# First products of two gated layers: seven products of quarter matrices instead of eight

## The chip, the cores and the metric

The kernel runs on one core of a Trainium2 chip. The time is the device time of one execution in microseconds (us), and the figure of a kernel is the median of its runs.

## What is computed

An attention over 8 batches, 8 heads, 576 positions and head size 64, whose softmaxes run over the features of q and over the positions of k, then two feed-forward layers over 4608 tokens of width 512:

```python
kv = np.einsum('bhsd,bhse->bhde', k_s, v)            # k_s: softmax over the positions
attn = np.einsum('bhsd,bhde->bhse', q_s, kv)         # q_s: softmax over the features
...
g = x @ w_gate                                       # 512 x 1536
silu = g * (1.0 / (1.0 + np.exp(-g)))
val = x @ w_val                                      # 512 x 1536
x = silu * val @ w_out                               # 1536 x 512
...
h = np.maximum(np.maximum(x @ w1, x @ w2), x @ w3)   # 512 x 768 each
out = h @ w_out                                      # 768 x 512
```

## The kernel before

Everything is float32 with a split: each operand is written as a high part in the type fp32r and the rest of it, and each product is made of three matmuls: high weights by high x, high weights by low x, low weights by high x. ScalarE makes the high part by a copy, and VectorE or GpSimd subtracts it from the original for the low part.

The 4608 tokens are nine blocks of 512. Layer 1 takes block after block, and in each the hidden width in 12 tiles of 128 (F1): a gate product into first_bank (12 matmuls of 512 columns: 4 pieces of the depth by 3), a value product into second_bank (12), and the second product of the tile before (L948 to L950, 12 matmuls), which adds up in four banks (acc_bank) over the whole block. Layer 2 has 6 tiles (F2) a block and three first products each (first_bank, second_bank, att_bank), then its second product (L965 to L967). ScalarE takes the tanh of the gate (L617) or a copy (L642), VectorE multiplies (L786, L796) or takes the maximum (L824, L830). `hidden` is then split: ScalarE writes h_hi (L556), VectorE h_lo (L693).

All weights of a layer stay in SBUF once split: 36 units of 128x512 for layer 1, read and split during the attention of batch 0 and block 0, and 24 for layer 2, during layer 1's last block. ScalarE makes the high part (L530), GpSimd the low one (L312). Apart from that GpSimd has little to do: the kv_lo split (L318) of each batch and, for batch 0, subtracting and scaling q (L325, L332).

Attention of a batch is 22 items of TensorE (ITEMS: transposed maxima KM, key-value products KV, transposed q QT, results X), each of a few matmuls into an att_bank. Batch 0 goes first; batch b + 1 is spread over block b of layer 1 by the table GAPS, one item in a gap between the 12-matmul products. VectorE does most of its elementwise work. A result goes to DRAM (x_dram) and comes back as the next blocks' x, and so do layer 1's results (x2_dram).

The order on each engine is written out by hand, and each engine takes its instructions strictly in turn; semaphores hold it where data isn't ready. Blocks in the middle run in hardware loops.

## Time and profile before

| | |
|---|---|
| median of 3 runs | 1600.42 us (1599.92 to 1603.34) |
| span of the profiled execution | 1598.4 us |
| TensorE busy | 1587.5 us, 7344 matmuls recorded |
| VectorE busy | 642.2 us |
| ScalarE busy | 399.3 us |
| GpSimd busy | 105.3 us, 115 instructions |
| DMA | 100.11 MB |

The span reaches from the first instruction to the last. A busy time is the time in which the engine had an instruction in work. A matmul's recorded duration is its latency, and the next one starts before it ends, so its cost is read from the distance of two starts. Some matmul records are missing from the trace. The layers follow each other: attention of batch 0 until about 43 us, layer 1 until about 1010 us, then layer 2.

### The profile page before, as it was taken

How to read it: one execution, taken by the hardware profiler on the slowest of the kernel's cores; microseconds unless marked ns; L12 is line 12 of the kernel's file. 1: busy time of each engine (PE TensorE's matmuls, PEld its weight loads, DVE VectorE, ACT ScalarE, POOL GpSimd, SP SyncE). 2: the span in 40 equal slices, each digit the busy share in tenths (PEclk: the TensorE clock that was granted, in tenths of full speed). 3: DMA queues.
4: the chain of work that ended last, by engine and by line, in shares of the span. 5: the costliest groups of instructions: out<-in, count | busy, mean ns of one | idle time of the engine just before them, and what ended most of it. 6: DMA issues, size and time to landing. Idle time of an engine off the chain costs nothing.

```text
span 1598.4 us, 19784 instructions
## 1 busy us (share of the span) xinstructions
PE 1587.5 (99%) x7344; PEld 1316.4 (82%) x7344; DVE 642.2 (40%) x1146; ACT 399.3 (25%) x753; POOL 105.3 (7%) x115
## 2 busy tenths in 40 slices
PE   8999999999999999999999999999999999999999
PEld 7888888888888888888888888888888888888887
DVE  6664654645645536546432322222322222222122
ACT  5543322313323223223121223211111112112111
POOL 5441000000000000000000034000000000000000
PEclk9999999999999999999999999999999999999999
DMA  8552312312223213122020032101101011010000
GB/s 232 171 149 85 100 50 82 89 61 78 62 71 90 64 52 103 50 75 59 30 79 1 17 108 73 53 1 53 52 0 52 0 52 52 0 52 30 23 26 27
DMA packets 81908, 100.11 MB, mean 63 GB/s; under 512 B 5968, under 2 KB 51024, under 8 KB 80720
## 3 DMA queue, kind: packets, MB, share of 16 engines
q1 hardware_dynamic: 73232, 83.91, 16.6%
q10 hardware_dynamic: 8640, 15.73, 3.4%
q8 instruction: 22, 0.36, 0.1%
q14 instruction: 14, 0.11, 0.0%
HBM read 71.30 MB, written 28.31 MB: 62 GB/s over the span
## 4 chain that ended last, share of the span: by engine, by line
PE 98%; DMA 1%; SPq 0%; DVE 0%; issue 0%; DVEq 0%
PE first_bank L870 10%; PE second_bank L870 9%; PE first_bank L872 9%; PE first_bank L871 9%; PE second_bank L872 9%; PE second_bank L871 9%; PE acc_bank L948 6%; PE acc_bank L950 6%; PE acc_bank L949 6%; PE acc_bank L966 3%; PE acc_bank L967 3%; PE acc_bank L965 3%; PE att_bank L871 3%; PE att_bank L870 3%; PE att_bank L872 3%; PE att_bank L921 2%
## 5 line engine op out<-in xcount | busy, mean ns | idle before, releaser
L556 ACT ACTIVATE h_hi<-hidden 128x512 fp32r<-128x512 f32 x161 | 101.7, 632 | 672.8 <-PE acc_bank L967 351.8
L693 DVE TENSOR_TENSOR h_lo<-hidden,h_hi 128x512 fp32r<-128x512 f32 x161 | 111.4, 692 | 388.9 <-ACT h_hi L556 388.9
L870 PE MATMUL first_bank<-x_hi,weights 128*128 128x512 f32 x644 | 254.6, 395 | 0.1
L870 PE MATMUL second_bank<-x_hi,weights 128*128 128x512 f32 x644 | 252.9, 393 | 0.0
L872 PE MATMUL first_bank<-x_hi,weights 128*128 128x512 f32 x644 | 251.1, 390 | 0.0
L871 PE MATMUL first_bank<-x_lo,weights 128*128 128x512 f32 x644 | 251.1, 390 | 0.0
L872 PE MATMUL second_bank<-x_hi,weights 128*128 128x512 f32 x644 | 250.9, 390 | 0.0
L871 PE MATMUL second_bank<-x_lo,weights 128*128 128x512 f32 x644 | 250.8, 389 | 0.0
L948 PE MATMUL acc_bank<-h_hi,weights 128*128 128x512 f32 x432 | 172.6, 399 | 0.0
L950 PE MATMUL acc_bank<-h_hi,weights 128*128 128x512 f32 x432 | 168.8, 391 | 0.0
L949 PE MATMUL acc_bank<-h_lo,weights 128*128 128x512 f32 x432 | 168.2, 389 | 0.0
L870 PEld LDWEIGHTS first_bank<-x_hi,weights 128*128 128x128 f32 x644 | 120.9, 188 | 27.0 <-issue 0.2
L872 PEld LDWEIGHTS first_bank<-x_hi,weights 128*128 128x128 f32 x644 | 120.8, 188 | 25.7
L872 PEld LDWEIGHTS second_bank<-x_hi,weights 128*128 128x128 f32 x644 | 120.8, 188 | 25.7
L871 PEld LDWEIGHTS second_bank<-x_lo,weights 128*128 128x128 f32 x644 | 121.1, 188 | 23.8
L870 PEld LDWEIGHTS second_bank<-x_hi,weights 128*128 128x128 f32 x644 | 121.0, 188 | 23.9
L871 PEld LDWEIGHTS first_bank<-x_lo,weights 128*128 128x128 f32 x644 | 120.9, 188 | 23.4
L786 DVE SCALAR_TENSOR_TENSOR hidden<-hidden,first_bank 128x512 f32<-128x512 f32 x108 | 73.9, 684 | 118.1 <-ACT hidden L617 117.6
L617 ACT ACTIVATE hidden<-first_bank 128x512 f32<-128x512 f32 x108 | 64.4, 596 | 226.8 <-PE first_bank L872 225.0
L824 DVE TENSOR_TENSOR hidden<-hidden,second_bank 128x512 f32<-128x512 f32 x54 | 37.1, 687 | 207.4 <-PE second_bank L872 207.4
L796 DVE SCALAR_TENSOR_TENSOR hidden<-hidden,second_bank 128x512 f32<-128x512 f32 x108 | 74.2, 687 | 93.6 <-PE second_bank L872 93.2
L950 PEld LDWEIGHTS acc_bank<-h_hi,weights 128*128 128x128 f32 x432 | 81.1, 188 | 17.9
(104 smaller groups left out, 1933.8 us busy)
## 6 DMA issues: line engine op xcount, KB each, us to landing
x_stage<-x_dram SPq DMA_DIRECT2D x17, 1024.0 KB, 5.3
w_stage<-w_l ACTq DMA_DIRECT2D x60, 256.0 KB, 2.7
x_dram<-x_stage SPq DMA_DIRECT2D x16, 576.0 KB, 3.4
x_dram<-result SPq DMA_DIRECT2D x36, 256.0 KB, 2.9
out<-result SPq DMA_DIRECT2D x36, 256.0 KB, 2.1
q_sb<-q SPq DMA_DIRECT2D x45, 192.0 KB, 2.4
kt_sb<-k_t SPq DMA_DIRECT2D x30, 288.0 KB, 2.9
k_sb<-k SPq DMA_DIRECT2D x30, 256.0 KB, 2.7
```

The costliest lines, as they stand in the source:

```text
L556: act.activation(split_tiles(very_last)[0], hidden[:, j % 2, :], ACT.Copy).then_inc(h_hi_ready, 1)
L617: act.activation(hidden[:, j % 2, :], first_bank[:, :], ACT.Tanh, scale=0.5)\
L693: dve.tensor_tensor(lo, hidden[:, j % 2, :], hi.bitcast(F32), ALU.subtract)\
L786: dve.scalar_tensor_tensor(out=hidden[:, j % 2, :], in0=hidden[:, j % 2, :], scalar=1.0, in1=first_bank[:, :], op0=ALU.add, op1=ALU.mult)\
L796: dve.scalar_tensor_tensor(out=hidden[:, j % 2, :], in0=hidden[:, j % 2, :], scalar=0.5, in1=second_bank[:, :], op0=ALU.mult, op1=ALU.mult)\
L870: pe.matmul(dst[:, :], weight(unit, 0, c), x_hi[:, c, :], start=(c == 0), stop=False)
L871: pe.matmul(dst[:, :], weight(unit, 0, c), x_lo[:, c, :], start=False, stop=False)
L872: mm = pe.matmul(dst[:, :], weight(unit, 1, c), x_hi[:, c, :], start=False, stop=(c == KT - 1))
L948: pe.matmul(acc_banks[m][:, :], weight(unit, 0, m), h_hi[:, :], start=(j == 0), stop=False)
L949: pe.matmul(acc_banks[m][:, :], weight(unit, 0, m), h_lo[:, :], start=False, stop=False)
L950: mm = pe.matmul(acc_banks[m][:, :], weight(unit, 1, m), h_hi[:, :], start=False, stop=last)
L965: pe.matmul(acc_banks[m][:, :], hi, weights[:, unit, 0, :], start=(j == 0), stop=False)
```

## The change

Block 0 of layer 1 stays as it was, but two batches (1 and 2) now run in it. The other eight blocks of layer 1 make four pairs; layer 2 takes the same eight blocks in four pairs and block 0 last, cut into two halves of 256 (so five pairs). For a pair of blocks, two tiles of the hidden width and one weight matrix (a group), the product of the 2x2 blocks of x and weights is made as seven products of quarters, each with half the depth (2 pieces by 3 matmuls), instead of eight. Their operands are sums and differences: of x once for a pair (sum_x, split_x: 7 operands of 128x1024), of the weights once for a group (combine_weights, split_weights: 4 combinations and 7 splits). The results C11, C12, C22 and C21 need sums too. Some are made in PSUM, since products add up in a bank, others take a copy of a bank to another (seed), a saved bank (save_p5, save_u2) and a sum on VectorE (add_c12, add_c22). Products are numbered in the order 1, 5, 2, 6, 3, 7, 4, and product 4 comes after product 1 of the next group.

A step is the two groups (gate, value) or three groups (the maxima) of two hidden tiles. Its second products are eight products of six matmuls (y_bank; four in the last pair), which VectorE adds up in SBUF (y_sb). They stand among the first products of the next step at the places in PLACES_8. The split weights no longer stay in SBUF: each group's are read, combined and split again for each pair (wring, two groups deep), and so are the output weights (wout). GpSimd makes the low parts of weights, output weights and the hidden tiles, and of three of the seven x operands. All loops are unrolled: whole_order() writes one list of events, and each engine goes through it; `at_once` is what an engine does at an event, `next_after` what it does one event later.

```diff
+SEVEN = (1, 5, 2, 6, 3, 7, 4)
...
+PLACES_8 = {1: [(0, 5), (0, 2), (0, 6), (0, 3), (1, 1), (1, 5), (1, 6)],
+            2: [(0, 5), (0, 6), (1, 1), (1, 5), (1, 6), (2, 1), (2, 6)]}
...
+    timed = spread(timed, (1, 2), 26)
...
+            for i in SEVEN:
+                if i == 4:
+                    continue
+                units.append(("product", n, i))
+                if i == 1 and kind == 0:
+                    units += carried
+                    carried = ys[-1:]
+                if ys and (kind, i) in places:
+                    units.append(ys[places.index((kind, i))])
+                if i == 1 and n:
+                    units.append(("product", n - 1, 4))
...
+            timed.append((where["product", final - 2, 6] + 0.3, ("load_x", pair + 1)))
+            timed.append((where["product", final - 1, 6] + 0.3, ("sum_x", pair + 1)))
+            for i in SEVEN[:-1]:
+                timed.append((where["product", final, i] + 1.4, ("split_x", pair + 1, X_OP[i])))
+        batches = [b for b in (3 + 2 * pair, 4 + 2 * pair) if b < BATCH] if pair < 3 else []
+        if batches:
+            timed = spread([(p, e) for p, e in timed], batches, 92)
...
         @block.gpsimd
...
+                    pool.tensor_tensor(combos[:, 0:2, :], of[:, 2:4, :],
+                                       of.rearrange("p (a b) e -> p a b e", b=2)[:, :, 0, :],
+                                       ALU.subtract).then_inc(combo_step, 1)
...
+                    pool.tensor_tensor(combos[:, 2, :], of[:, 3, :], combos[:, 0, :], ALU.subtract)\
...
+                    pool.tensor_tensor(combos[:, 3, :], of[:, 1, :], combos[:, 2, :], ALU.subtract)\
...
+            def split_wout(s, f):
+                slot = (2 * s + f) % 4
+                pool.wait_ge(wout_hi, 2 * s + f + 1)
...
+            def split_h(s, t):
+                cols = STEPS[s].cols
+                pool.wait_ge(h_hi_ready, 4 * s + ORDER[t] + 1)
...
+                elif e[0] == "product":
+                    _, n, i = e
+                    if i in (2, 6, 3, 7) and n + 1 < NGROUPS:
+                        split_weights(n + 1, (2, 6, 3, 7).index(i))
+                    if i == 4 and n + 2 < NGROUPS:
+                        combine_weights(n + 2, (0, 1, 2))
...
+                    if closer(n) and i in TILE:
+                        split_h(GROUPS[n].step, TILE[i])
+                    if GROUPS[n].kind == 1 and i in (3, 7):
+                        split_wout(GROUPS[n].step, (3, 7).index(i))
...
         @block.scalar
...
+            def save_u2(n):
+                cols = GROUPS[n].cols
+                act.wait_ge(done[6], n + 1)
+                if n:
+                    act.wait_ge(c12_ready, n)
+                act.activation(u2[:, 0:cols], b_bank(n)[:, 0:cols], ACT.Copy).then_inc(u2_saved, 1)
...
         @block.vector
...
+            def add_c22(n):
+                g = GROUPS[n]
+                dve.wait_ge(done[7], n + 1)
+                dve.wait_ge(p5_saved, n + 1)
...
         @block.tensor
...
+                for c in range(2):
+                    hi, lo = of[:, 0, c * P:(c + 1) * P], of[:, 1, c * P:(c + 1) * P]
+                    x1, x2 = xops[:, o, 0, c, 0:g.cols], xops[:, o, 1, c, 0:g.cols]
+                    pe.matmul(dst[:, 0:g.cols], hi, x1, start=(i in (1, 5) and c == 0), stop=False,
+                              skip_group_check=True)
+                    pe.matmul(dst[:, 0:g.cols], hi, x2, start=False, stop=False, skip_group_check=True)
+                    mm = pe.matmul(dst[:, 0:g.cols], lo, x1, start=False, stop=(c == 1), skip_group_check=True)
...
+            def second_product(s, unit):
...
+                t, m = divmod(unit, step.units // 2)
+                pe.wait_ge(h_lo_ready, 4 * s + (2 if t == 0 else 4))
+                pe.wait_ge(wout_lo, 2 * s + 2)
```

On GpSimd, before: block 0's last weights (weights), the loop over the kv_lo splits of batches 2 to 7, which is all that GpSimd does in the blocks of layer 1 between, in its order.

```order
L312 TENSOR_TENSOR weights<-w_stage,weights 128x512 [waits w_hi_ready] x12
L354 UNCONDITIONAL_BRANCH
L354 ISA
L318 TENSOR_TENSOR kv_lo<-kv,kv_hi 128x128 [waits kv_hi_ready]
L317 REGISTER_ALU
```

After, the end of one step of layer 1: the value group (wring are the next gate group's weights, h the step's hidden tiles, wout its output weights).

```order
L495 TENSOR_TENSOR wring<-raw,wring 128x2x256 [waits w_hi]
L500 TENSOR_TENSOR wring<-combos,wring 128x2x256 [waits w_hi]
L516 TENSOR_TENSOR h<-hid,h 128x512 [waits h_hi_ready]
L500 TENSOR_TENSOR wring<-combos,wring 128x2x256 [waits w_hi]
L504 TENSOR_TENSOR wring<-raw,wring 128x256 [waits w_hi]
L516 TENSOR_TENSOR h<-hid,h 128x512 [waits h_hi_ready]
L510 TENSOR_TENSOR wout<-wraw,wout 128x512 [waits wout_hi]
L516 TENSOR_TENSOR h<-hid,h 128x512 [waits h_hi_ready]
L510 TENSOR_TENSOR wout<-wraw,wout 128x512 [waits wout_hi]
L479 TENSOR_TENSOR combos<-raw 128x512 [waits w_lo,raw_in1]
```

The low parts of the hidden tiles came from VectorE, and weights were split once; both are now in GpSimd's turn, the output weights last.

On TensorE, before, a second product of layer 1 after a value product:

```order
L871 MATMUL second_bank<-x_lo,weights 128x512
L872 MATMUL second_bank<-x_hi,weights 128x512
L948 MATMUL acc_bank<-h_hi,weights 128x512 [waits h_lo_ready]
L949 MATMUL acc_bank<-h_lo,weights 128x512
L950 MATMUL acc_bank<-h_hi,weights 128x512
```

After, the gate group's product 5 and the first second product of the step before:

```order
L1381 MATMUL third_bank<-xops,wring 128x512 [waits w_lo,h_ready]
L1383 MATMUL third_bank<-xops,wring 128x512
L1384 MATMUL third_bank<-xops,wring 128x512
L1381 MATMUL third_bank<-xops,wring 128x512
L1383 MATMUL third_bank<-xops,wring 128x512
L1384 MATMUL third_bank<-xops,wring 128x512
L1406 MATMUL y_bank<-h,wout 128x512 [waits wout_lo,h_lo_ready,y_taken]
L1407 MATMUL y_bank<-h,wout 128x512
```

A product is six matmuls instead of twelve, and the second product now waits for wout_lo and h_lo_ready, which both come from GpSimd.

On ScalarE, before: layer 1's last block (hidden is the gate, h_hi the split of the tile, weights a unit of layer 2).

```order
L617 ACTIVATE hidden<-first_bank 128x512 [waits gate_done,h_lo_ready]
L515 DMA w_stage<-w_l 128x512 [waits w_lo_ready]
L530 ACTIVATE weights<-w_stage 128x512 [waits w_in0,val_done]
L556 ACTIVATE h_hi<-hidden 128x512 [waits h_used,hidden_ready]
L515 DMA w_stage<-w_l 128x512 [waits w_lo_ready]
L530 ACTIVATE weights<-w_stage 128x512 [waits w_in1,val_done]
```

After, the value group of a step of layer 1 (p and u are the saved banks of products 5 and 6).

```order
L842 ACTIVATE p<-third_bank 128x512 [waits c22_ready,product5_done]
L900 ACTIVATE wring<-raw 128x2x256 [waits raw_in0,product4_done]
L849 ACTIVATE u<-round 128x512 [waits c12_ready,product6_done]
L890 ACTIVATE h<-hid 128x512 [waits y_done,h_ready]
L903 ACTIVATE wring<-combos 128x4x256 [waits combo_step]
L905 ACTIVATE wring<-raw 128x256
L890 ACTIVATE h<-hid 128x512 [waits y_done,h_ready]
L914 ACTIVATE wout<-wraw 128x512 [waits wraw_in,y_done]
```

The high part of the combinations, which GpSimd's second weight piece needs, stands behind the saving of product 6 and a hidden tile.

At the end of a pair of layer 2, on GpSimd after the change (the last group: x operands, xops, stand between the weights):

```order
L479 TENSOR_TENSOR combos<-raw 128x512 [waits w_lo,raw_in1]
L484 TENSOR_TENSOR combos<-raw,combos 128x256 [waits combo_step]
L488 TENSOR_TENSOR combos<-raw,combos 128x256 [waits combo_step]
L495 TENSOR_TENSOR wring<-raw,wring 128x2x256 [waits w_hi]
L516 TENSOR_TENSOR h<-hid,h 128x512 [waits h_hi_ready]
L500 TENSOR_TENSOR wring<-combos,wring 128x2x256 [waits w_hi]
L532 TENSOR_TENSOR xops<-stage,xops 128x1024 [waits op_hi]
L500 TENSOR_TENSOR wring<-combos,wring 128x2x256 [waits w_hi]
L532 TENSOR_TENSOR xops<-stage,xops 128x1024 [waits op_hi]
L504 TENSOR_TENSOR wring<-raw,wring 128x256 [waits w_hi]
L516 TENSOR_TENSOR h<-hid,h 128x512 [waits h_hi_ready] x2
L532 TENSOR_TENSOR xops<-stage,xops 128x1024 [waits op_hi]
```

Here GpSimd of the kernel before had nothing to do: all its work is new.

## Rows read from the trace of the kernel before

**Rows 1.** The page: busy time by engine, then the chain that ended last.

```profile
PE 1587.5 (99%) x7344; PEld 1316.4 (82%) x7344; DVE 642.2 (40%) x1146; ACT 399.3 (25%) x753; POOL 105.3 (7%) x115
...
PE 98%; DMA 1%; SPq 0%; DVE 0%; issue 0%; DVEq 0%
```

**Rows 2.** Timeline of TensorE in layer 1: start and duration (us), first and thirteenth matmul.

```profile
800.58 0.39 PE L870 MATMUL first_bank<-x_hi,weights 128*128 128x512 f32 x1
...
803.30 0.39 PE L870 MATMUL second_bank<-x_hi,weights 128*128 128x512 f32 x1
```

**Rows 3.** Timeline of TensorE, matmuls of 256 columns, the first and the seventeenth.

```profile
41.37 0.28 PE L889 MATMUL first_bank<-x_lo,weights 128*128 128x256 f32 x1
...
43.27 0.28 PE L890 MATMUL second_bank<-x_hi,weights 128*128 128x256 f32 x1
```

**Rows 4.** GpSimd's groups by line: xcount | busy us, mean ns | idle before us.

```profile
L312 POOL TENSOR_TENSOR weights<-w_stage,weights 128x512 fp32r<-128x512 f32 x60 | 77.4, 1290 | 257.5 <-ACT weights L530 257.5
L318 POOL TENSOR_TENSOR kv_lo<-kv,kv_hi 128x128 fp32r<-128x128 f32 x32 | 14.8, 462 | 619.3 <-ACT kv_hi L597 619.3
L332 POOL TENSOR_TENSOR q_sb<-q_sb,q_rec 96x512 f32<-96x512 f32 x3 | 3.1, 1041 | 3.2 <-DVE q_rec L732 3.2
```

**Rows 5.** Timeline of GpSimd: a wait for itself, a split at the start, two in a row.

```profile
1.19 0.29 POOL L301 TENSOR_SCALAR_AFFINE_SELECT ident<-ident 128x128 f32<-128x128 f32 x1 [0.24 <-POOL ident L299]
...
12.62 1.27 POOL L312 TENSOR_TENSOR weights<-w_stage,weights 128x512 fp32r<-128x512 f32 x1 [1.54 <-ACT weights L530]
...
989.75 2.54 POOL L312 TENSOR_TENSOR weights<-w_stage,weights 128x512 fp32r<-128x512 f32 x2 [1.94 <-ACT weights L530]
```

**Rows 6.** ScalarE's groups by line.

```profile
L556 ACT ACTIVATE h_hi<-hidden 128x512 fp32r<-128x512 f32 x161 | 101.7, 632 | 672.8 <-PE acc_bank L967 351.8 <-PE acc_bank L950 319.8 <-DVE hidden L796 1.1
L617 ACT ACTIVATE hidden<-first_bank 128x512 f32<-128x512 f32 x108 | 64.4, 596 | 226.8 <-PE first_bank L872 225.0 <-PE first_bank L890 1.8
...
L597 ACT ACTIVATE kv_hi<-kv 128x128 fp32r<-128x128 f32 x32 | 10.0, 311 | 2.9
```

**Rows 7.** VectorE's groups by line.

```profile
L693 DVE TENSOR_TENSOR h_lo<-hidden,h_hi 128x512 fp32r<-128x512 f32 x161 | 111.4, 692 | 388.9 <-ACT h_hi L556 388.9
L796 DVE SCALAR_TENSOR_TENSOR hidden<-hidden,second_bank 128x512 f32<-128x512 f32 x108 | 74.2, 687 | 93.6 <-PE second_bank L872 93.2 <-PE second_bank L890 0.2
```

**Rows 8.** Timeline in layer 2: a product's last matmul and VectorE after it.

```profile
1151.23 0.39 PE L872 MATMUL second_bank<-x_hi,weights 128*128 128x512 f32 x1
...
1151.66 0.69 DVE L824 TENSOR_TENSOR hidden<-hidden,second_bank 128x512 f32<-128x512 f32 x1 [2.88 <-PE second_bank L872]
```

**Rows 9.** Timeline: ScalarE's split of a weight and GpSimd's after it.

```profile
36.20 0.63 ACT L530 ACTIVATE weights<-w_stage 128x512 fp32r<-128x512 f32 x1 [0.37 <-POOL weights L312]
...
36.91 1.28 POOL L312 TENSOR_TENSOR weights<-w_stage,weights 128x512 fp32r<-128x512 f32 x1 [1.12 <-ACT weights L530]
```

**Rows 10.** Timeline of GpSimd: the same split of two batches, one block apart.

```profile
397.78 0.46 POOL L318 TENSOR_TENSOR kv_lo<-kv,kv_hi 128x128 fp32r<-128x128 f32 x1 [79.37 <-ACT kv_hi L597]
...
508.23 0.46 POOL L318 TENSOR_TENSOR kv_lo<-kv,kv_hi 128x128 fp32r<-128x128 f32 x1 [79.37 <-ACT kv_hi L597]
```

**Rows 11.** Stretches: length, busy us of each engine, granted clock, DMA share, GB/s.

```profile
core 0: us, PE busy (x) PEld busy (x) DVE busy (x) ACT busy (x) POOL busy (x), PEclk, DMA share, GB/s
0.00:40.00 40.00, 33.43 (x226) 30.34 (x226) 27.20 (x65) 20.32 (x47) 21.82 (x33) 0.96 0.85 232
230.00:340.00 110.00, 110.00 (x524) 91.03 (x523) 58.57 (x112) 30.90 (x62) 1.85 (x4) 1.00 0.24 73
780.00:890.00 110.00, 110.00 (x491) 91.24 (x491) 33.10 (x51) 20.00 (x33) 0.00 (x0) 1.00 0.11 35
890.00:990.00 100.00, 100.00 (x443) 82.81 (x442) 29.20 (x43) 31.99 (x55) 28.61 (x23) 1.00 0.26 79
```

1282 lines of the change are left out of this document (829 added, 453 removed).

## The prediction

> **What bounds the kernel now.** I read the page's busy totals and its chain of waits first: TensorE is busy 1587.5 of 1598.4 us and 98% of the chain is its own work, so only fewer or cheaper matmuls, or new waits, can move the time [rows 1]. Then I priced a matmul. The listed 390 ns is a latency with overlap; what counts is the distance between starts. Twelve matmuls of 512 columns go from 800.58 to 803.30 us: 0.227 us each, so six of them, the size of one product of the new kernel (a "unit" below), take 1.36 us [rows 2]. Sixteen steps of 256 columns take 1.90 us: 0.119 us each [rows 3]. Third, the other engines, because the change gives them work: GpSimd is busy 7% of the span, VectorE 40%, ScalarE 25% [rows 1].
>
> **What the change removes.** A group (2 tiles of the hidden width, 2 token blocks) takes 42 matmuls instead of 48. Layer 1 has 48 groups, layer 2 has 36 full ones: 84 x 6 = 504 fewer. The last pair is one block of 512 cut in two halves: 9 x 42 = 378 matmuls of 256 columns (45.0 us) for 216 of 512 (49.0 us). Block 0 and the second products keep their number. Saved: 504 x 0.227 + 4.0 = 118.2 us. With nothing else this is a span of 1480.2 us.
>
> **What it adds.** For each group GpSimd now forms four weight combinations and splits seven weight pieces, and for each step it splits four hidden tiles and two output weights. Its prices: 1.29 us for 128x512, 0.46 us for 128x128 [rows 4], so 2.16 ns per further element; two back to back take 2.54 us, so one in a row costs 1.25 us [rows 5]. That makes 256 elements 0.70 and 1024 elements 2.36 (estimates from these). An instruction that waits for the one before it on GpSimd loses 0.24 us [rows 5]. The combinations are plain float32, and the nearest float32 row, 1.04 us for 96x512 with a broadcast operand, would make them a fifth cheaper; I take 1.25 because their operands are both full, as in the splits. Combining: 1.25 + 2 x 0.70 + 2 x 0.24 = 3.1; splitting: 3 x 1.25 + 0.70 = 4.5; a group 7.6 us. A step of layer 1 is 22 units, 29.9 us of TensorE, and 2 x 7.6 + 6 x 1.25 = 22.7 us of GpSimd (76%); a step of layer 2 is 29 units, 39.4 us, against 30.3 us (77%). So GpSimd isn't short on average. Its order decides, since it takes everything in turn.
>
> ScalarE: 0.60 us from PSUM, 0.63 from SBUF [rows 6], 1.06 for 1024 elements (0.31 for 128 gives the slope): about 14 of 29.9 us. VectorE: 20 instructions of 0.69 [rows 7], 13.8 of 29.9 us. A copy from PSUM to PSUM and a sum into PSUM stand in no row; 0.55 to 0.70 us bounds them, and they have two units of cover. Hand-overs: TensorE's last matmul starts at 1151.23 and VectorE at 1151.66, 0.20 us after the unit's end [rows 8]; ScalarE ends at 36.83 and GpSimd starts at 36.91, 0.08 us [rows 9].
>
> **Layer 1, end of every step.** The value group's product 6 ends; ScalarE saves U2 (0.20 + 0.60), splits hidden tile 0 (0.63) and the combinations (1.06), GpSimd starts 0.08 later: 2.6 us. From there GpSimd runs without a gap through two weight pieces, hidden tile 0 between them, the short piece, hidden 1, output weight 0, hidden 3, output weight 1: 7 x 1.25 + 0.70 = 9.5, ready at 12.0 us. The first second product of the step waits for output weight 1 and stands seven units behind: 9.5 us. TensorE waits 2.5 us. Behind it on TensorE stands everything. With attention between the units the gap narrows: 12.5 us of attention matmuls (a block with a batch lasts 110.45 us [rows 10], 432 x 0.227 = 97.9) over 46 units give 1.9 us in seven units, and GpSimd and ScalarE get some work too: I take 1.3 us of wait; with one batch for a whole pair 1.8. At the end of a pair a 2.36 us operand split stands in the same run, and VectorE delays C22: 5.3 us. Sum: 8 x 1.3 + 4 x 1.8 + 8 x 2.5 (five in pair 3, one each in pairs 0, 1, 2) + 4 x 5.3 = 59 us. The bounds are 35 (no wait beside attention, 4 at the ends) and 75.
>
> **Layer 2.** In a plain step the second product needs only hidden 0 and 1, and output weights were split a group earlier: GpSimd is 1.3 us early, no wait. At the end of a pair it isn't. Its run begins when the middle group's product 6 is saved (17 units + 1.9 = 25.1 us into the step) and holds, up to the first weight piece of the next pair's second group, 12 x 1.25, 2 x 0.70, the three sums of x (3 x 2.36 + 0.5 = 7.6), three operand splits (7.1) and two combinings (6.3): 37.4, so 62.5 us, where TensorE wants it at 39 units, 53.0. Lost: 9.4 us, three times, 28 us (bounds 15 and 36).
>
> **Last pair.** At 256 columns TensorE's work shrinks, the weights' doesn't: 21 x 0.714 + 8 x 1.36, then twice 21 x 0.714 + 4 x 1.36, 66.7 us for three steps. GpSimd from its last operand split (50.0 us into the step before) has 8 x 3.1, 8 x 4.45, 6 x 1.25 and the hidden splits (7): 75 us, so its last weights come at 125 where TensorE's need for them is at 104. With the products that queue behind the first piece I take 23 us (15 to 30).
>
> **Attention.** Two batches now share block 0, in 26 twelve-matmul places: 26 x 2.72 + 25 = 96 us. VectorE has 58.57 us in a stretch of 110 us with a batch and 33.10 without [rows 11]; scaled to the blocks a batch costs it 29 us. Block 0's places thus hold 58 + 18 = 76 us of VectorE, two thirds of a batch's share in the first half of its time (maxima, four of six q tiles): about 23 us of work in 23 us, taken in strict turn with ScalarE. The first 40 us, where a batch runs that closely, show the DMA 85% busy, TensorE 33.4 busy [rows 11]. I take 13 us (3 to 30), and 2 for the first pair's operands. In pairs 0 and 1 VectorE again has some 36 us in 36: 3 us for each of four batches, 12 us (3 to 25).
>
> **Sum.** 1480.2 + 59 + 28 + 23 + 15 + 12 = 1617 us of span. The profiled execution is 2.0 us under the median of 1600.4, so 1619 us: slower by 1%, since the waits (137) outweigh the matmuls (118).
>
> A rule of the skill bears on this. A 128x512 subtraction takes GpSimd 1.29 us and VectorE 0.69 [rows 4, 7]. The Trainium skill (GPSIMD Engine Reference, Performance versus the Vector engine) puts elementwise work on VectorE, GpSimd being about half as fast with two inputs. By that rule the trace agrees, and it speaks against where this change puts the weights.
>
> **Rivals.**
> (a) TensorE keeps most of the saving: attention hides in VectorE's slack and GpSimd's runs are a fifth shorter (the 1.04 us row [rows 4]). Waits of 35 + 15 + 15 + 5 + 3 = 73: 1555 us. Against it: the layer 1 run is counted from rows, and only combinations could be cheaper, which it doesn't hold. Partly so, it ends near 1580. For it: nothing in those runs is allowed to be late but the named ones.
> (b) GpSimd is ahead everywhere, full saving: 1482 us. It would need splits below 1.0 us; no row shows one.
> (c) VectorE becomes the bound beside attention: each C22 it delivers late stops TensorE (two units of cover, 2.7 us, 0.9 used). It decides from a lag of 1.8 us, which three queued instructions make. All upper bounds: 75 + 36 + 30 + 32 + 25 = 198: 1680 us; half way 1650.
> (d) VectorE and GpSimd get in each other's way. GpSimd's split takes 1.27 us in the first 40 us, with VectorE 68% busy, and two take 2.54 us near 990 us, with it 29% busy [rows 5, 11], so no. Would each q subtraction and scaling hold GpSimd for its 0.69 us, 12 a batch over five batches, at most 41 us came on top: 1660 us. The Trainium skill (GPSIMD Engine Reference, the overview's table) says the two share SBUF interfaces, with contention from VectorE instructions that have two SBUF inputs; the trace does not show it.
> (e) The clock falls with the waits. It was 0.96 in the first 40 us, with TensorE 33.4 busy [rows 11], and the waits here are far sparser; were it 0.96 throughout layer 1, 0.04 x 780 = 31 us more.
> That the matmuls aren't removed is excluded by the instruction order.
>
> **How the numbers follow.** Forecast 0.42 (1597 to 1640), (a) 0.32, (b) 0.03, (c) 0.15, (d) 0.05, (e) 0.03. Cases below 1570 and above 1665 hold about 2 in 10. A measurement can tell 0.2% (3.2 us) from no change. Faster: (a) and (b), and a little of the forecast's lower edge, 0.36; within 0.2%: 0.08, from the edge between forecast and (a); slower 0.56.
>
> **What would show it.** Right: TensorE idle about 2.5 us before the y_bank products once per step where there is no attention, released by GpSimd's wout; 9 us around pair ends of layer 2; GpSimd near 100% in the last 80 us; splits still 1.29 us. A group's first products 9.5 us per 42 matmuls. Wrong: y_bank products without waits in pair 3, combinations well under 1.2 us, or waits on c22 or attention items above 30 us in all.

## The result

The changed kernel takes **1747.62 us** (median of 4 runs, 1736.93 to 1751.78) where the kernel before takes 1600.17 us (4 runs on the same chip, 1598.44 to 1603.34): a ratio of 1.091, 95% interval [1.087, 1.094]. The forecast was 1619 us with a range of 1570 to 1665. The direction was right, the size was not: of 129 us that are missing, none is in the matmuls. The profiled execution took 1751.78 us, its span is 1750.0.

The page of the changed kernel answers to [rows 1]: busy time by engine, the clock that TensorE was granted in 40 slices (tenths of full speed), the share of each engine in the chain that ended last.

```profile
span 1750.0 us, 21089 instructions
PE 1558.6 (89%) x7002; PEld 1271.3 (73%) x7002; DVE 940.8 (54%) x1437; ACT 718.5 (41%) x1308; POOL 1225.4 (70%) x1030
PEclk9888989999999999999998999899999999999999
PE 55%; POOL 25%; DVE 9%; issue 6%; ACT 4%; DMA 1%; SPq 0%; ACTq 0%; DVEq 0%; POOLq 0%
```

There are 342 matmuls fewer (7344 to 7002), as counted. But TensorE's own work is 55% of the chain, not 98%, and it is busy for 1558.6 us, 89 more than the 1469.3 that 1587.5 less 118.2 would give, because part of the matmuls run at the lower clock: the mean granted clock is 0.95, where the kernel before had 1.00 from 42 us on.

Three groups of instructions of VectorE and GpSimd from the changed kernel (by line: count | busy us, mean ns | idle before) answer to [rows 4, 7]:

```profile
L1142 DVE SCALAR_TENSOR_TENSOR hid<-hid,round 128x512 f32<-128x512 f32 x48 | 32.8, 684 | 19.4 <-PE round L1384 19.3
L1142 DVE SCALAR_TENSOR_TENSOR hid<-hid,c 128x512 f32<-128x512 f32 x24 | 32.3, 1344 | 0.1
L500 POOL TENSOR_TENSOR wring<-combos,wring 128x512 fp32r<-128x512 f32 x186 | 253.6, 1375 | 120.6 <-ACT wring L903 120.6
```

The first two are the same operation on the same number of elements. One reads its tile from PSUM (round) and takes 0.684 us, the other from SBUF (c, the tile C22) and takes 1.344.

**One step of layer 1 without attention.** This is the place on which the largest term of the prediction rests. First GpSimd's run behind the value group's product 6, from its first combination to the last output weight; then TensorE at the first second product of the step (start us, us).

```profile
981.59 1.29 POOL L500 TENSOR_TENSOR wring<-combos,wring 128x512 fp32r<-128x512 f32 x1 [3.74 <-ACT wring L903]
...
985.35 1.18 POOL L504 TENSOR_TENSOR wring<-raw,wring 128x256 fp32r<-128x256 f32 x1
...
990.22 1.27 POOL L510 TENSOR_TENSOR wout<-wraw,wout 128x512 fp32r<-128x512 f32 x1
```

```profile
988.54 0.39 PE L1384 MATMUL third_bank<-xops,wring 128*128 128x512 f32 x1
991.63 0.76 PE L1406 MATMUL y_bank<-h,wout 128*128 128x512 f32 x1 [2.70 <-POOL wout L510]
992.19 0.63 PE L1407 MATMUL y_bank<-h,wout 128*128 128x512 f32 x1
992.62 0.63 PE L1408 MATMUL y_bank<-h,wout 128*128 128x512 f32 x1
...
995.04 0.40 PE L1384 MATMUL round<-xops,wring 128*128 128x512 f32 x1
```

The run takes 9.9 us where 9.5 was forecast (the short piece at 985.35 takes 1.18 us and not 0.73: VectorE's C22 operation lies beside it), and TensorE waits 2.70 us where 2.5 was forecast. Then comes what the forecast did not have: the matmuls start 0.43 us apart, not 0.23. Stretches around it (length, busy us of each engine, granted clock, DMA share, GB/s):

```profile
984.00:988.90 4.90, 4.90 (x22) 3.75 (x20) 3.31 (x5) 2.71 (x5) 4.90 (x5) 1.00 0.27 73
988.90:991.60 2.70, 0.02 (x1) 0.00 (x1) 0.00 (x0) 1.63 (x3) 2.70 (x4) 0.97 0.15 62
991.60:995.30 3.70, 3.67 (x10) 2.93 (x11) 0.69 (x1) 0.00 (x0) 3.54 (x4) 0.56 0.43 142
995.30:1000.00 4.70, 4.70 (x22) 3.89 (x21) 1.28 (x2) 2.45 (x4) 3.68 (x4) 1.00 0.02 5
```

The clock is 1.00 before, 0.56 in the 3.7 us behind the pause (that is mostly the lower level, 1.2 GHz) and 1.00 again. A step without attention takes 34.5 us instead of 29.9: 2.7 us of pause and 1.9 us of slow work.

**Where the 270 us stand.** I cut the span at product 5 of each pair's first group and took off the matmul time that the prediction has for each stretch (1480.2 us in all, of which 1469.3 are TensorE's work and 10.9 the idle time that the kernel before has too). What is over, in us, for the changed kernel and for the kernels of the experiments below:

| over the matmul time in | forecast | changed | exp. 1: GpSimd an eighth | exp. 2: wout early | exp. 6: x early | exp. 7: h on VectorE | exp. 9: split once | exp. 11: best |
|---|---|---|---|---|---|---|---|---|
| block 0 and entry | 15 | 72 | 65 | 61 | 58 | 61 | 62 | 62 |
| layer 1, pairs 0 to 3 | 71 | 121 | 26 | 62 | 60 | 66 | 36 | 29 |
| layer 2, three full pairs | 28 | 49 | 2 | 43 | 23 | 15 | 16 | 13 |
| layer 2, the rest | 23 | 28 | 4 | 30 | 24 | 16 | 4 | 6 |
| sum | 137 | 270 | 97 | 197 | 165 | 158 | 118 | 110 |

Every stage is over its forecast, block 0 by the most: 57 of the 133 us between 137 and 270, layer 1's pairs 50, the full pairs of layer 2 21, the rest 5.

The first row needs care. Block 0 has the same program in the changed kernel and in experiments 1, 2, 3, 6, 7, 9 and 10, and still ends at 234.3 us in the changed kernel's profiled execution and between 219.3 and 226.9 in theirs. So what a change outside block 0 is worth is read from the other rows; 7 to 15 us of each difference to the changed kernel's profiled execution stand in block 0 and are not the change's doing.

### The profile page after: what moved, and what is told of

It reads as the page before. It is cut to its first block, busy times and chain, and to the rows that moved or that the text cites. A ratio compares the mean times of both kernels' runs of the same rounds, so it can differ in the third digit from the quotient of the medians.

```text
span 1750.0 us, 21089 instructions
## 1 busy us (share of the span) xinstructions
PE 1558.6 (89%) x7002; PEld 1271.3 (73%) x7002; DVE 940.8 (54%) x1437; ACT 718.5 (41%) x1308; POOL 1225.4 (70%) x1030
## 4 chain that ended last, share of the span: by engine, by line
PE 55%; POOL 25%; DVE 9%; issue 6%; ACT 4%; DMA 1%; SPq 0%; ACTq 0%; DVEq 0%; POOLq 0%
PE round L1381 8%; PE round L1383 7%; PE round L1384 7%; PE y_bank L1406 6%; PE y_bank L1408 6%; PE y_bank L1407 5%; POOL h L516 5%; POOL wring L500 5%; POOL wout L510 4%; PE third_bank L1381 3%; PE third_bank L1384 3%; PE third_bank L1383 3%; POOL xops L532 2%; PE att_bank L1319 2%; POOL combos L479 1%
## 5 line engine op out<-in xcount | busy, mean ns | idle before, releaser
L1381 PE MATMUL round<-xops,wring 128*128 128x512 f32 (+1 forms) x930 | 367.9, 396 | 53.4 <-DVE c L1116 17.3
L1383 PE MATMUL round<-xops,wring 128*128 128x512 f32 (+1 forms) x930 | 360.1, 387 | 0.0
L1384 PE MATMUL round<-xops,wring 128*128 128x512 f32 (+1 forms) x930 | 359.3, 386 | 0.0
L1181 DVE TENSOR_TENSOR y_sb<-y_sb,y_bank 128x512 f32<-128x512 f32 x232 | 159.1, 686 | 362.5 <-PE y_bank L1408 361.8
L500 POOL TENSOR_TENSOR wring<-combos,wring 128x512 fp32r<-128x512 f32 x186 | 253.6, 1375 | 120.6 <-ACT wring L903 120.6
L1381 PEld LDWEIGHTS round<-xops,wring 128*128 128x128 f32 x930 | 180.6, 194 | 99.3 <-DVE c L1116 22.0
L516 POOL TENSOR_TENSOR h<-hid,h 128x512 fp32r<-128x512 f32 (+1 forms) x156 | 211.2, 1358 | 34.6 <-ACT h L890 34.5
L1406 PE MATMUL y_bank<-h,wout 128*128 128x512 f32 x384 | 160.3, 418 | 66.1 <-POOL wout L510 66.0
L495 POOL TENSOR_TENSOR wring<-raw,wring 128x512 fp32r<-128x512 f32 x93 | 122.7, 1319 | 123.7 <-ACT wring L900 123.6
L1384 PEld LDWEIGHTS round<-xops,wring 128*128 128x128 f32 x930 | 179.7, 193 | 35.4
L1383 PEld LDWEIGHTS round<-xops,wring 128*128 128x128 f32 x930 | 180.7, 194 | 32.5
L1408 PE MATMUL y_bank<-h,wout 128*128 128x512 f32 x384 | 157.3, 410 | 0.0
L1407 PE MATMUL y_bank<-h,wout 128*128 128x512 f32 x384 | 156.8, 408 | 0.0
L1381 PE MATMUL third_bank<-xops,wring 128*128 128x512 f32 (+1 forms) x372 | 143.6, 386 | 0.0
L1383 PE MATMUL third_bank<-xops,wring 128*128 128x512 f32 (+1 forms) x372 | 142.2, 382 | 0.0
L1384 PE MATMUL third_bank<-xops,wring 128*128 128x512 f32 (+1 forms) x372 | 142.1, 382 | 0.0
L479 POOL TENSOR_TENSOR combos<-raw 128x512 f32<-128x512 f32 x93 | 124.7, 1341 | 6.9 <-DMA raw<-w_g 6.9
L510 POOL TENSOR_TENSOR wout<-wraw,wout 128x512 fp32r<-128x512 f32 x78 | 103.6, 1332 | 4.1 <-ACT wout L914 4.1
```

Of the source, the lines that this page charges most:

```text
L479: pool.tensor_tensor(combos[:, 0:2, :], of[:, 2:4, :], of.rearrange("p (a b) e -> p a b e", b=2)[:, :, 0, :], ALU.subtract).then_inc(combo ...
L495: pool.tensor_tensor(to[:, 0:2, 1, :], of[:, 0:2, :], to[:, 0:2, 0, :].bitcast(F32), ALU.subtract).then_inc(w_lo, 1)
L500: pool.tensor_tensor(to[:, a + 1:a + 3, 1, :], combos[:, a - 2:a, :], to[:, a + 1:a + 3, 0, :].bitcast(F32), ALU.subtract).then_inc(w_lo, 1)
L510: pool.tensor_tensor(wout[:, slot, 1, :], wraw[:, f, :], wout[:, slot, 0, :].bitcast(F32), ALU.subtract).then_inc(wout_lo, 1)
L516: pool.tensor_tensor(h[:, t, 1, 0:cols], hid[:, t, 0:cols], h[:, t, 0, 0:cols].bitcast(F32), ALU.subtract).then_inc(h_lo_ready, 1)
L1181: dve.tensor_tensor(to, to, src, ALU.add).then_inc(y_taken, 1)
```

## The experiments

My theory after the traces: GpSimd's order makes the pauses, as predicted, and three things that I had small or at nothing are added: the clock behind each pause, contention between VectorE and GpSimd, and block 0. Rivals: the quarter products have a slower pitch of their own; the low clock belongs to the load as a whole and not to pauses; VectorE's long operations come from their tiles and not from GpSimd.

### 1. GpSimd's work on an eighth of the columns

```
-                    pool.tensor_tensor(combos[:, 0:2, :], of[:, 2:4, :],
+                    pool.tensor_tensor(combos[:, 0:2, 0:w], of[:, 2:4, 0:w],
...
-                cols = STEPS[s].cols
+                cols = 64 if s else STEPS[s].cols
```

> The changed kernel with GpSimd's work of the pairs (combinations, splits of weights, operands and hidden tiles) done on an eighth of the columns from the second step on; the low parts and combinations then hold stale numbers, TensorE's instructions are all the same. If the 270 us above the matmul time come from GpSimd's length (its run of 8 operations after the last combination took 12 us against 9.5 us of cover) and from what follows such waits, the pause at y_bank line 1406 goes, a layer-1 step takes 29.9 us (now 34.5) and the three pair ends of layer 2 lose their 15 to 20 us each: some 1747 - 100 - 60 = about 1590 us, with block 0 (72 us over) left as it is. Second question, contention: hid<-hid,c on VectorE (two SBUF inputs, 1.34 us) falls back to about 0.69 us, the PSUM-source forms stay at 0.68 to 0.69. Rival (quarter products themselves pitch slower than the pattern): the layer-1 step stays above 33 us and the time above 1700.

Measured: 1577.67 us (1590 expected), 0.986 [0.984, 0.988] of the kernel before. A step is 29.9 us, three full pairs of layer 2 lose 2 us together, and the operation on C22 is back at its length (line 1145 here is line 1142 above; the same columns):

```profile
L1145 DVE SCALAR_TENSOR_TENSOR hid<-hid,c 128x512 f32<-128x512 f32 x24 | 16.9, 702 | 0.1
```

So 166 of the 198 us that the changed kernel is over outside block 0 come from GpSimd: its length, what it does to VectorE, and the clock behind the pauses. The clock's part can be bounded. Worked out from the granted clock outside block 0, the lower level stands for 107 us in the changed kernel, with TensorE busy in 89 of them, and for 6 us here, with TensorE busy in 3: half of 86, at most 43 us, is work done at half speed. VectorE is busy for 851.7 us instead of 940.8 with the same 1437 instructions: 89 us less, which is what GpSimd's length added to VectorE's work; how much of it TensorE waited for isn't separated. The rival of a slower pitch falls. The saving of 118 us in matmuls is real, and 97 us of loss, 65 of them in block 0, don't hang on GpSimd's length in the pairs.

### 2. Output weights split one group earlier

```
-                    if GROUPS[n].kind == 1 and i in (3, 7):
+                    if GROUPS[n].kind == GROUPS[n].layer - 1 and i in (3, 7):
                         split_wout(GROUPS[n].step, (3, 7).index(i))
```

The loads and ScalarE's splits of these weights move with GpSimd's.

> The changed kernel with one thing moved: in layer 1 the output weights are loaded and split during the gate group, not the value group, on ScalarE, GpSimd and the queue of SP. The value group's GpSimd run ahead of hidden 0 is then two operations (2 x 1.3 us) shorter: 9.4 us against 9.5 us of cover. Waits theory: the pause at y_bank line 1406 (2.70 us) goes in the steps without attention, and with it the 1.9 us per step of half clock behind it: 4.6 us for each of about 20 steps, 1747 - 92 = about 1655 us. Rival (the low clock comes from the load of the run as a whole and not from the pauses): only the pauses go, 2.7 x 20 = 54, about 1693 us, and the clock stays at a mean of 0.95. Rival (GpSimd is the limit of the step anyway, the pause moves to another product): within 15 us of 1747.

Measured: 1677.58 us (1671.7 to 1686.0), 1.049 [1.045, 1.053] of the kernel before: 70 us less than the changed kernel. By the table 59 of them are in layer 1, where the change is; 11 are block 0, whose program is the same. A step without attention takes 13.6 + 16.3 us, exactly its matmul time, and no pause stands at y_bank there. One place in the order was worth 59 us. The expectations (92 and 54 us) bracket it; the mean clock rose from 0.95 to 0.965, where the rival had it stay. Experiments 3 and 4 decide between them. The changed kernel had 21 waits for the output weight, 66.0 us in all. They went, and in part others came in their place: C22 from VectorE 25.4 us (17.3 before), and ahead of the second products, mostly at pair ends, 11.7 us in 5 waits of which the profile doesn't tell the cause (2.9 in one before).

### 3. Matmuls in the pause

```
+                if step.layer == 1 and unit == 0 and not step.final:
+                    for _ in range(9):
+                        pe.matmul(dst[:, :], fill, xops[:, X_OP[2], 0, 0, :], start=True, stop=True,
+                                  skip_group_check=True)
```

> The changed kernel with work added only: nine matmuls of 512 columns whose result is overwritten stand on TensorE ahead of the first second product of each layer-1 step, so that they lie in the pause at y_bank line 1406. They need nothing that is late. Nine at 0.227 us are 2.05 us of the 2.70 us pause. If the half clock (0.56 from 991.6 to 995.3 us) follows from the pause, the clock stays at 1.0 there and the kernel gets faster though it does more: up to 1.9 x 23 steps = 44 us, about 1705 us. If the clock doesn't hang on the pause: 1747 or a few us more (fillers issued where there was no pause cost up to 2 us each).

Measured: 1730.37 us, 17 us faster than the changed kernel although it does 2 us of work more in each of 20 steps (180 matmuls more; the last step of each pair has none). Its timeline at one of these places, then the stretches before, across and behind it:

```profile
1007.59 2.20 PE L1398 MATMUL y_bank<-xops,wring 128*128 128x512 f32 x9
1010.49 0.47 PE L1411 MATMUL y_bank<-h,wout 128*128 128x512 f32 x1 [0.70 <-POOL wout L510]
1010.80 0.40 PE L1412 MATMUL y_bank<-h,wout 128*128 128x512 f32 x1
```

```profile
1004.00:1008.00 4.00, 4.00 (x19) 3.34 (x18) 2.14 (x3) 2.59 (x6) 4.00 (x5) 1.00 0.40 124
1008.00:1010.40 2.40, 1.79 (x8) 1.13 (x7) 0.00 (x0) 1.42 (x3) 2.40 (x3) 1.00 0.05 19
1010.40:1014.00 3.60, 3.51 (x16) 2.94 (x17) 0.69 (x1) 0.44 (x1) 3.44 (x4) 1.00 0.47 146
```

The wait for GpSimd is the same, but TensorE is idle for 0.70 us of it, and the clock stays at 1.00. A step goes from 34.5 to 32.9 us: 1.6 of the 1.9 expected. That is the finding; the 17 us in all are not, because in the two traces block 0, where nothing changed, is 13 us shorter. The four pairs of layer 1 take 887.5 instead of 893.4 us: pairs 2 and 3 are 6 us shorter each, and pairs 0 and 1 are 3 us longer each. In seven of the ten places there the changed kernel's wait was under 1.5 us or none, so the fillers were in the way.

### 4. The clock's price by itself

The kernel before, with 16 pauses in layer 2 of which TensorE waits for one or two GpSimd operations.

```
+                for j in (1, 4):
+                    pool.wait_ge(w1_done, F2 * i + j + 1)
+                    for k in range(2):
+                        sub = pool.tensor_tensor(weights[:, 34 + k, 1, :], ...)
+                    sub.then_inc(extra, 1)
...
+                    if not first and j in (1, 4):
+                        pe.wait_ge(extra, 2 * (i - 1) + (1, 4).index(j) + 1)
                     product(second_bank, 4 * j + 1, BLOCKS + i).then_inc(w2_done, 1)
```

> The kernel before with nothing changed but 16 pauses: twice in each of the last eight blocks of layer 2, TensorE waits after the first product of a step until GpSimd, which starts on the end of that product, has done two subtractions of 128 x 512 (2.6 us). Nothing else hangs on it. The pauses alone are 16 x 2.8 = 45 us: 1645 us. If each is followed by the 1.9 us that the changed kernel lost at half clock behind its pause of 2.70 us, 1675 us, and the windows behind the pauses show a granted clock near 0.56.

> The same with one subtraction (1.3 us) for each of the 16 pauses. Pauses alone: 16 x 1.5 = 24 us, 1624 us. If the clock falls after short pauses as after long ones, 30 us more, 1654 us; if it falls by the length of the pause, something under 1640 us.

Measured: 1670.33 us with the long pauses and 1628.46 with the short ones, over 1599.88 of the kernel before in the same session: 4.40 and 1.79 us for each pause. TensorE's timeline at one pause of each, the long first:

```profile
1160.83 0.50 PE L878 MATMUL second_bank<-x_hi,weights 128*128 128x512 f32 x1 [2.68 <-POOL weights L363]
1161.16 0.40 PE L879 MATMUL second_bank<-x_lo,weights 128*128 128x512 f32 x1
...
1162.66 0.63 PE L878 MATMUL second_bank<-x_hi,weights 128*128 128x512 f32 x1
1163.09 0.63 PE L879 MATMUL second_bank<-x_lo,weights 128*128 128x512 f32 x1
```

```profile
1189.46 0.50 PE L878 MATMUL second_bank<-x_hi,weights 128*128 128x512 f32 x1 [1.46 <-POOL weights L363]
...
1191.19 0.39 PE L879 MATMUL second_bank<-x_lo,weights 128*128 128x512 f32 x1
1191.42 0.40 PE L880 MATMUL second_bank<-x_hi,weights 128*128 128x512 f32 x1
```

Behind the long pause eight matmuls start 0.43 us apart. I took the starts around all 32 pauses: the long ones open a gap of 2.84 us, and the next 24 matmuls take 1.76 us too long in 14 of 16 cases, 0.15 in the other two. The eight begin at once in some cases and up to six matmuls later in others; what decides that, and why two pauses went free, these runs don't show. 14 x 4.60 + 2 x 2.99 = 70.4 us, the measured difference. The short ones open 1.62 us and the next 24 matmuls take 0.15 too long in all 16: 28.3 us, measured 28.6. So a pause of 2.8 us costs 4.6, one of 1.6 us costs 1.8, and the low clock follows the pause, not the load of the run as a whole. The changed kernel's pauses open 2.87 us each, in the costly kind.

### 5. Contention by itself

The kernel before, with 400 GpSimd subtractions that nothing waits for.

```
+            for k in range(400):
+                if k:
+                    pool.wait_ge(extra, k)
+                pool.tensor_tensor(weights[:, 35, 1, :], weights[:, 34, 0, :].bitcast(F32),
+                                   weights[:, 35, 0, :].bitcast(F32), ALU.subtract).then_inc(extra, 1)
```

> The kernel before with 400 GpSimd subtractions (128 x 512, one after another, into weight slots that layer 2 doesn't use) added behind its own splits of layer 2; nothing waits for them. It asks what GpSimd at work does to VectorE with nothing else changed. Contention theory: h_lo (line 693, both inputs in SBUF, 0.692 us) rises to about 1.3 us while GpSimd is busy, the VectorE forms with a PSUM input (line 796, 0.687 us) stay, and a GpSimd operation takes 1.35 to 1.45 us instead of 1.29. Rival (VectorE's length in the changed kernel comes from its wider or strided tiles): line 693 stays at 0.69 us. The time: the kernel before has slack on VectorE in layer 2, so 1600 to 1615 us either way.

Measured: 1608.09 us, 1.005 [1.003, 1.007]. The groups of GpSimd's new line and of a VectorE form with a PSUM input, then single h_lo operations (two SBUF inputs) while GpSimd runs:

```profile
L363 POOL TENSOR_TENSOR weights<-weights 128x512 fp32r<-128x512 f32 x400 | 544.2, 1360 | 54.7 <-PE acc_bank L956 23.4
L836 DVE TENSOR_TENSOR hidden<-hidden,att_bank 128x512 f32<-128x512 f32 x54 | 37.0, 686 | 96.3 <-PE att_bank L878 96.3
```

```profile
1159.68 0.69 DVE L699 TENSOR_TENSOR h_lo<-hidden,h_hi 128x512 fp32r<-128x512 f32 x1 [2.69 <-ACT h_hi L562]
1170.56 1.07 DVE L699 TENSOR_TENSOR h_lo<-hidden,h_hi 128x512 fp32r<-128x512 f32 x1 [2.69 <-ACT h_hi L562]
1181.44 1.46 DVE L699 TENSOR_TENSOR h_lo<-hidden,h_hi 128x512 fp32r<-128x512 f32 x1 [2.69 <-ACT h_hi L562]
1192.32 1.81 DVE L699 TENSOR_TENSOR h_lo<-hidden,h_hi 128x512 fp32r<-128x512 f32 x1 [2.69 <-ACT h_hi L562]
```

The operation takes 0.69 us plus anything up to 1.1. That is what is left of the GpSimd operation that had begun: in layer 2 all 41 h_lo operations that took longer than 0.75 us end 0.55 us after the end of a GpSimd operation that had started before them. In the kernel before the same 161 operations took 0.692 us each [rows 7]. The PSUM form stays at 0.686. GpSimd's own 400 operations take 1.36 us instead of 1.29. So the long VectorE operations of the changed kernel are contention, not a matter of their tiles. It reaches TensorE where VectorE has no slack: of the 8 us that this kernel is longer, 4.9 are eight waits of TensorE for x_lo, VectorE's split with two SBUF inputs, which took 1.58 us (mean in layer 2) instead of 0.69. The Trainium skill (SBUF — State Buffer, Who interferes with whom) says that whoever starts first holds the shared pair for the whole instruction and the other is fully blocked, and counts VectorE instructions with two SBUF inputs among those that need it; by that rule the trace agrees, with 0.69 to 1.81 us beside GpSimd and 0.69 alone.

### 6. Layer 2: x one step earlier

```
+            early = 4 if pair >= PAIRS1 else 0
-                timed.append((where["product", final - 2, 6] + 0.3, ("load_x", pair + 1)))
+                timed.append((where["product", final - 2 - early, 6] + 0.3, ("load_x", pair + 1)))
```

> As the kernel with the output weights in the gate group (1677.6 us), and in layer 2 the next pair's x is loaded and summed one step (three groups or more) earlier. There each pair end costs 14.4 us (groups of 23.1 and 17.1 us where the steady ones take 12.2 and 13.6): GpSimd has three x sums of 2.4 us and the sixteen operations of two groups in the same stretch. If GpSimd's queue at that place is the cause, 9 to 14 us go at each of three pair ends and some at the entry of layer 2 and of the last pair: 1635 to 1645 us. Rival (the operands' splits, which stay where they are, are what is late, or their ring buffers): under 10 us in all, above 1667 us.

Measured: 1648.96 us, 29 us less than experiment 2. The three full pairs go from 14.4 to 7.5 us over their matmul time, the last part from 30 to 24. So half of each pair end came from the place of x, its load and its three sums, in GpSimd's order; the other half stays.

### 7. Low parts of the hidden tiles on VectorE

```
-                    if closer(n) and i in TILE:
-                        split_h(GROUPS[n].step, TILE[i])
...
+            def split_h(s, t):
+                dve.wait_ge(h_hi_ready, 4 * s + ORDER[t] + 1)
+                dve.tensor_tensor(h[:, t, 1, 0:cols], hid[:, t, 0:cols], h[:, t, 0, 0:cols].bitcast(F32), ...)
```

> As the kernel before it in this call, and the low parts of the hidden tiles (four 128 x 512 subtractions in a step, 1.38 us each) are made on VectorE, not on GpSimd. GpSimd's length as the cause: the steps beside attention (groups of 17 to 22 us) lose what they have over the run with GpSimd at an eighth, 15 to 25 us in pairs 0 to 2, and the last pair, where GpSimd had eleven operations for every 31 us of products, 5 to 10: 1605 to 1620 us. Rival (VectorE is by now as long, its two-input forms stretched to 1.3 us by GpSimd, and the second products wait for it): no gain or 5 to 15 us slower than the kernel before it in this call.

Measured: 1637.79 us, 11 us less, where I expected 29 to 44. It helped where there is no attention (layer 2: 23 to 15 us, the last part 24 to 16) and hurt beside it: pair 0 goes from 19 to 25 us over, pair 1 from 23 to 25. That fits both theories, each in its place: beside attention VectorE is nearly as short of time as GpSimd. No run takes VectorE's work away in pairs 0 and 1, so this is argued.

### 8. Block 0: clock and density

```
+                if b in (1, 2) and n not in (13, 14, 19, 20, 21):
+                    for _ in range(3):
+                        pe.matmul(dst[:, :], x_hi[:, 0, 0:P], x_hi[:, 0, :], start=True, stop=True)
```

> As the kernel before it in this call, and ahead of 34 attention items beside block 0 stand three extra matmuls of 512 columns each (0.68 us at full clock) whose result is overwritten. In the changed kernel that stretch (43 to 230 us) had TensorE busy for 143 us at a mean clock of 0.85. If the low clock is half of the loss there, the clock goes to above 0.95 and the first pair starts 5 to 15 us sooner, though 23 us of work are added: 10 us below the kernel before it. Rival (the attention's round trips alone set that stretch, and what TensorE does between them costs nothing and gives nothing): the start stays within 3 us. Rival (the fillers stand in front of items that were ready): up to 23 us slower.

Measured: 1642.57 us. Between 43 and 204 us the granted clock went from 0.92 to 0.97 and TensorE's busy time from 127.8 to 141.3 us, and the first pair started at 225.0 instead of 223.4 us. With the clock restored the stretch is as long. That doesn't prove that the clock costs nothing there, since 13.5 us of busy time were added; it shows that fillers between round trips buy nothing.

```
-    timed = spread(timed, (1, 2), 26)
+    timed = [(p - 1.5, e) for p, e in spread([], (1, 2), 30)] + timed
```

> As the kernel with the low parts of the hidden tiles on VectorE (1637.8 us), and the attention of the two batches beside block 0 is spread over 30 units instead of 26 and begins 1.5 units earlier. In the changed kernel 44 attention items in 26 units wait for each other's round trips, 57 us or more lost between 43 and 230 us. If their density is the cause, the first pair starts 8 to 15 us sooner than at 223 us: 1623 to 1630 us. Rival (the entry decides: x of the second batch is now ready later, and the load of the first pair's operands, its sums and splits follow it): the start stays or comes up to 8 us later, 1638 to 1646 us.

Measured: 1657.92 us. The first pair starts at 241.2 us, 18 us later: more than the rival's 8. The waits for k_max are 27.1 us in all instead of 15.1. Spreading the attention wider doesn't buy time; that the rest of the 18 us is x, which is ready later, is argued.

### 9. Weights combined and split once in a layer

The first pair of each layer makes the seven matrices, stores them to DRAM, and the later pairs read them back into the ring, piece by piece as products free their places. It stands on experiment 6; made(n) numbers the group whose matrices group n uses.

```
+            def store_split(n):
+                sp.wait_ge(w_lo, 4 * made(n) + 4)
+                sp.dma_start(w_split[made(n)], wring[:, n % 2, :, :, :].bitcast(F32)).then_inc(wst[n % 2], 16)
+
+            def load_piece(n, i):
+                sp.wait_ge(done[i], n - 1)
...
+                sp.dma_start(wring[:, n % 2, W_OP[i], :, :].bitcast(F32), w_split[made(n), :, W_OP[i], :, :])\
+                  .then_inc(piece_in[n % 2][i], 16)
```

> As the kernel with x one step early (1649.0 us), and the seven weight matrices of a group, high and low parts, are made once in each layer (first pair), stored to DRAM and read back in the later pairs, straight into the weights' ring, instead of combined and split anew by GpSimd and ScalarE. GpSimd keeps the output weights, the hidden tiles and x. GpSimd's length as the cause of what is left outside block 0: the pairs that read back come to what they had with GpSimd at an eighth (22.6 to 13 and 9.9 to 3 us over in pairs 1 and 2, 8.4 to 3 in pair 3, 7 to 1 in each pair of layer 2 but the first, 20 to 5 in the last): 50 to 60 us, 1590 to 1600 us. Rival (DMA takes its place): each group then reads 1.84 MB, 144 GB/s in layer 2 where the changed kernel moved 0.5 MB; the highest rate in the traces' windows is 155 GB/s at a share of 0.52. If the pieces land late TensorE waits for them in every group, 1650 us or more.

Measured: 1599.98 us (10 runs, 1598.2 to 1604.3), 1.000 [0.999, 1.001] of the kernel before, and 49 us less than experiment 6 (50 to 60 expected). From its page, its DMA issues, and a stretch of 95 us in layer 2:

```profile
PE 1508.0 (94%) x7002; PEld 1241.0 (78%) x7002; DVE 915.1 (57%) x1437; ACT 589.8 (37%) x1092; POOL 681.3 (43%) x526
wring<-w_split SPq DMA_DIRECT2D x504, 256.0 KB, 2.9
1290.00:1385.00 95.00, 95.00 (x421) 78.65 (x420) 35.65 (x54) 22.75 (x40) 23.90 (x16) 1.00 0.65 197
```

GpSimd's 1225 us are 681, TensorE is busy 95.00 of 95.00 us at 197 GB/s of DMA, and no wait on a piece stands in the list of waits. Reading prepared weights again is cheaper here than preparing them again. 197 GB/s is above the 155 GB/s that I had taken as the highest seen (wrongly: the kernel before has 232 in its first 40 us [rows 11]), and did no harm.

### 10. The difference of x parts on GpSimd

In the trace of experiment 9, VectorE at a pair end of layer 2, where TensorE waits 2.63 us for C22:

```profile
1393.50 2.85 DVE L1227 TENSOR_TENSOR xops<-stage,xops 128x1024 fp32r<-128x1024 f32 x1
1396.45 3.22 DVE L1233 TENSOR_TENSOR stage<-stage 128x1024 f32<-128x1024 f32 x1
1399.60 0.69 DVE L1144 TENSOR_TENSOR third_bank<-third_bank,u 128x512 f32<-128x512 f32 x1
1400.20 0.68 DVE L1157 TENSOR_TENSOR c<-round,p 128x512 f32<-128x512 f32 x1
```

```
-                if o == 2:
+                if o == 2 and pair == 0:
...
+                if o == 3 and pair:
+                    pool.tensor_tensor(stage[:, 2, :, 0:cols], stage[:, 2, :, 0:cols], stage[:, 3, :, 0:cols], ...)
```

> As the kernel that splits the weights once in a layer (1600.0 us), and in all pairs but the first the difference of x parts for product 3 (line 1233 there, 128 x 1024, both inputs in SBUF) is made by GpSimd, not VectorE. In the trace of that kernel VectorE is held by it for 3.22 us (1396.45) and by the operand split ahead of it for 2.85 us while GpSimd also works, the sum for C22 follows only at 1400.20, and TensorE waits 2.63 us at round line 1424 and runs on at half clock: 4.5 us at each pair end of layer 2. Contention and VectorE's order as the cause: 3 to 4.5 us less at seven pair ends, 1571 to 1580 us. Rival (the operand split of 2.85 us alone is enough to hold it, or GpSimd's own splits come late instead): under 8 us in all.

Measured: 1594.25 us, 6 us less, where I expected 20 to 29. The wait for C22 went, and at the same place TensorE now waits 1.71 us ahead of a second product: a group of 16.1 us where 13.6 would do. At the layer-2 pair ends the last group goes from 16.2 to 12.2 us and the first of the next pair from 14.1 to 16.1: the next wait in line took half of the gain. Of the 6 us in all, 5 are block 0, where nothing changed; outside it the two traces differ by 2 us, and the ranges (1598.2 to 1604.3 and 1587.6 to 1598.1) nearly touch.

### 11. Entry of the first pair

```
+        raw_first = y_sb[:, 4:8, :].rearrange("p (g a) (b e) -> p g (a b) e", g=2, b=2)
...
-                elif e[0] == "gate" and e[1] == 10:
+                elif e[0] == "gate" and e[1] == 4:
```

> As the kernel before it in this call, and the raw weights of the first two groups are loaded some 15 units earlier into a free part of another buffer and combined three units earlier, so that the first pair doesn't wait for a load that GpSimd waited 7.4 us for and TensorE 6.3 us. If that load sets the first pair's entry, the pair starts 5 to 9 us sooner (now 224.0 us): 1565 to 1575 us. Rival (x, its sums of 2.4 us each and the splits behind them are as late as the weights): under 3 us.

Measured: 1587.95 us (4 runs, 1582.0 to 1592.2), 0.991 [0.989, 0.993] of the kernel before. TensorE's wait of 6.6 us at the first pair's product is gone (the one at block 0's last second product is 3.1 us, 2.3 before), and pair 0 has 14 instead of 21 us over; its start isn't earlier in this execution (224.2 us), since block 0 itself ran at a clock of 0.85 here and 0.93 in the trace of experiment 10. The expected start can't be read there. The median is 6 us under experiment 10, where 5 to 9 was expected, but the two ranges overlap and the traces are 2 us apart, so the gain isn't clear of noise; that the wait went is. The expected 1565 to 1575 us counted on experiment 10's full gain.

### 12. Leads, and the length of the attention steps

```
+    lead = {"max_k": 1.0, "max_q": 1.0, "exp_q": 0.7, "sum_q": 0.4}
+    timed += [(p - lead.get(e[0], 0), e) for p, e in spread([], (1, 2), 26)]
```

> As the kernel before it in this call, and beside block 0 VectorE and ScalarE take their attention steps (maximum of k and q, exp, sum) 0.4 to 1.0 unit earlier in their order against TensorE's items. The two batches there stand in 26 units instead of 72, and the leads in the order shrank with them. If the leads set the loss that neither the clock (fillers) nor the density (wider spread) explained, the waits on k_max and on q go (about 10 us between 43 and 210 us) and with them half clock behind them: 6 to 15 us sooner. Rival (the loads of k and q, one buffer each, or the two PSUM banks set it): within 3 us.

Measured: 1588.10 us, no change. The waits for k_max went from 7.7 to 1.8 us between 43 and 200 us, and waits for k_sb from ScalarE of 5.2 and 5.5 us came in their place.

The last kernel stands on experiment 11; one of its edits, of which ScalarE's and VectorE's other attention steps have the like:

```
+                w = 8 if (b in (1, 2)) else HD
+                dve.tensor_tensor(tile[:, :, 0:w], tile[:, :, 0:w], ...)
```

> As the kernel with the first weights early (1588.0 us), and the vector and scalar steps of the attention of the two batches beside block 0 (maxima, subtractions, exp, sums, scalings, splits, copies) on an eighth of their columns; their x is then not what it should be. TensorE's instructions and all orders stay. If the length of these steps, in strict turn with TensorE's items, makes the stretch from 43 to 224 us, TensorE's waits there (33 us over 1.2 us each) mostly go and the first pair starts at 185 to 205 us, 20 to 40 us sooner: 1550 to 1568 us. Rival (loads of k, q and v through few buffers, and the queue of SP): the start stays above 215 us.

Measured: 1563.44 us, and the first pair starts at 197.6 instead of 224.2 us, inside the expected 185 to 205. Both kernels from 43 to 190 us, this one first (columns as above):

```profile
43.00:190.00 147.00, 127.72 (x586) 103.08 (x586) 66.25 (x177) 48.23 (x122) 56.79 (x46) 0.93 0.50 156
```

```profile
43.00:190.00 147.00, 112.68 (x475) 88.88 (x474) 85.21 (x166) 51.20 (x109) 41.20 (x38) 0.84 0.45 136
```

With the steps short, TensorE's waits of over 1.2 us ahead of the first pair fall from 33 to 19 us, and 27 us of block 0's 62 go; by the medians of the whole kernels it is 24.5. So the length of VectorE's and ScalarE's steps, in turn with TensorE's attention items, makes about 25 of them, with what the clock lost behind their waits. 35 us stay, of which 19 are those waits and some 10 the clock (0.93 over 147 us: 20 us at the lower level); the rest is open.

## Why the prediction was wrong, point by point

Two steps failed most. Block 0 was priced from an average of VectorE's work: 15 us with the entry, and 72 measured. And the clock stands in the sum with nothing, where up to 73 us were lost to it, 29 of them inside block 0's 72. GpSimd's pauses, the mechanism that the forecast rested on, came as described. Of the prediction's own signs of being wrong one came: waits on C22 (17.3 us) and on attention items (32 us between 43 and 200 us alone) are above 30 us in all.

**Matmuls saved, 118.2 us.** Right. Steps without a pause take 13.6 + 16.3 us, and with GpSimd shortened two full pairs of layer 2 take 118.5 and 118.4 us for 118.3.

**GpSimd's prices and its order.** Right: 1.28 to 1.30 us alone, a run of 9.9 us for 9.5, a pause of 2.70 for 2.5, at the named instruction. The waits for the output weight are 66.0 us in 21 places where the term has 59 in 24; the four pair ends were too small, 7.4 us for 5.3. GpSimd was the main loss (experiment 1). That experiment 2 took 59 us out of layer 1 is not the term come true: it holds the clock behind the pauses, less the waits that came instead.

**The clock, rival (e): the step that failed most clearly.** The sum has nothing for it. I wrote that waits here are far sparser than in the first 40 us and so priced the clock at 31 us with a chance of 0.03. Sparse waits lower it as well: experiment 4 shows 1.76 us behind a pause of 2.84 us in 14 of 16 cases, each 37 us from the next. At a mean clock of 0.95 a tenth of the 1750 us ran at the lower level, 175 us; TensorE was busy for 146 of them, so up to 73 us were lost, 29 of them in block 0 and 30 in layer 1's pairs. The first 40 us were the wrong row for it. The sum should have added 1.8 us behind each of its pauses of 2.5 us and more, which stood in it one by one: 21 us for the twelve in layer 1 alone.

**Contention, rival (d), chance 0.05.** The mechanism is real and I had excluded it by the wrong rows: they show GpSimd's length, and the delay was VectorE's. The row that would have spoken is one of VectorE's smallest operations, here twice from the kernel before:

```profile
8.35 0.17 DVE L730 TENSOR_SCALAR q_sum_eps<-q_sum 96x8 f32<-96x8 f32 x1
...
13.27 0.66 DVE L730 TENSOR_SCALAR q_sum_eps<-q_sum 96x8 f32<-96x8 f32 x1
```

The second began while GpSimd's split of 12.62 to 13.89 us ran [rows 5] and ended 0.03 us after it; nine of the 48 are long in this way, and each ends 0.02 to 0.03 us after a GpSimd operation. I called the contention bounded by 41 us. VectorE alone was busy 89 us longer by it (experiment 1); its share of the 166 us that hang on GpSimd isn't separated by these runs. Experiment 5 shows its size for one operation (0.69 to 1.81 us), experiment 10 that taking one 3.22 us operation out gives 2 us outside block 0.

**Block 0, 13 us (bounds 3 to 30).** Mis-sized, the largest error of the sum, and no bound held: 58 to 72, with 2 forecast for the first pair's operands. I divided VectorE's work by the time and took what was over. But two batches in strict turn pay each hand-over (15 waits of 1.2 to 3.2 us each between 43 and 200 us, 32 us in all), and an average over 23 us of work doesn't show them. Experiment 12 names about 25 us of it, and some 10 are the clock; filling matmuls, a wider spread and leads were each tried and gave nothing (experiments 8 and 12). The rest is open.

**Ends of layer-2 pairs, 9.4 us each.** The place was right; 14 to 20 measured. VectorE's operand splits of 128 x 1024 took 2.05 us beside GpSimd and 1.39 with GpSimd short, its x difference 2.53, and the clock fell behind the pauses: over the three pairs it stood at the lower level for 21 us, with TensorE busy in 16.

**The last pair, 23 us.** 28 with the end of the pair before it (7): inside its bounds.

**The sum and the chances.** Five cases were priced as rivals of each other. They are not exclusive: the changed kernel has the forecast's pauses, (d) and (e) at once, and probably (c)'s shortage of VectorE beside attention (experiment 7). A range from their single prices ended at 1665; added up (1617 + 41 + 31, and block 0's upper bound of 17 more) they give 1706. Of the 44 us that are still missing from the span of 1750, 40 are block 0 beyond its bound, some 10 of these by an execution in which its clock was low. That "slower" came true says little: the forecast had 1% and a chance of 0.56 for it.

## What to carry to other kernels

Saving TensorE's work by giving 23 to 30 us of every 30 to 39 to a slower engine is decided by the order on that engine: splitting the output weights one group earlier was worth 59 us. Price a pause of TensorE with what the clock costs behind it, here 4.6 us for 2.8 and 1.8 for 1.6, and where a pause comes regularly and can't be avoided, matmuls that fill it keep the clock (1.6 us for a step); where there is no such pause they cost time. And work that repeats with the same data (here the weights' combinations and splits) is better read back than made again while the DMA has room: that turned 1649 into 1600 us, and with two more changes of place 1588, 0.9% under the kernel before.

## What the runs showed of the hardware

- A VectorE operation with two SBUF inputs waits for the end of a GpSimd operation that has begun: 0.69 us became 0.69 to 1.81 in experiment 5 and up to 2.33 in the changed kernel, mean 1.34 for line 1142. With one input from PSUM the same operation took 0.67 to 0.69 us, every time. It works both ways: a GpSimd operation of 0.73 us took 1.18, and one of 1.29 took up to 2.3. A VectorE operation of 96x8 with one input waited too: 0.17 us alone, up to 0.66 in the kernel before and 1.29 in the changed one.
- The clock follows single pauses: after 2.84 us of idle TensorE eight matmuls ran 0.43 us apart in 14 of 16 cases, after 1.62 us in none of 16, and nine filling matmuls in a wait for GpSimd kept it at 1.00.
- The same instructions take different times where the clock moves: block 0 is the same program in several of these kernels, and the first pair started between 219.3 and 226.9 us, with a granted clock of 0.84 to 0.89 from 43 to 120 us and 0.91 to 0.96 up to 200; the changed kernel's profiled execution, the longest of its four, had 0.84 and 0.83 there and 234.3 us. About 10 of its 72 us are this.
